# Order of VectorE's work at the group borders: turns of weights and logits ahead of the next unit's first scan

## What is computed

```python
for t in range(S):                                   # attention with a decaying state
    cur = einsum('bhd,bhe->bhde', u[None] * kt, vt)
    y[:, :, t] = einsum('bhd,bhde->bhe', rt, state + cur)
    state = wt[:, :, :, None] * state + einsum('bhd,bhe->bhde', kt, vt)

h = x @ w_in                                         # gated layer, 384 -> 2048 -> 384
x = (h * clip(h + 3, 0, 6) / 6) @ w_out

logits = x @ phi                                     # soft mixture, 32 slots, 8 experts
d = softmax of logits over the tokens;  slot_input = d.T @ x
slot_out = relu(slot_input @ w1[e]) @ w2[e]
out = (softmax of logits over the slots) @ slot_out
```

## Time and profile before

| | |
|---|---|
| median of three runs | 419.66 us (419.65 to 419.80) |
| the profiled execution's own time | 419.48 us |
| its span, first to last instruction | 417.8 us |
| granted TensorE clock, mean | 0.991 |
| PE busy | 400.4 us, 96% |
| DVE busy | 342.0 us, 82% |
| POOL busy | 187.7 us, 45% |
| ACT busy | 162.6 us, 39% |

### The profile page before, as it was taken

How to read it: one execution, slowest core, us unless ns; L and a number is a source line. 1 busy time by engine, 2 the same in 40 slices (tenths; PEclk the granted TensorE clock), 3 DMA queues, 4 the chain that set the end, 5 groups by cost and what they waited for, 6 DMA issues and landing times.

```text
span 417.8 us, 9795 instructions
## 1 busy us (share of the span) xinstructions
PE 400.4 (96%) x3913; PEld 219.5 (53%) x3913; DVE 342.0 (82%) x566; ACT 162.6 (39%) x300; POOL 187.7 (45%) x178
## 2 busy tenths in 40 slices
PE   8999999999999999999999999999999999999981
PEld 3885555555555555565554556445453444544430
DVE  7998799999998889999989998989975887662152
ACT  3586256533343245144433434351333234321141
POOL 4445988865465755445653556564450012010000
PEclk9999999999999999999999999999999999999996
DMA  8998321468033124314430321331006199779929
GB/s 246 336 404 296 125 90 36 124 238 296 17 124 119 60 70 126 91 36 124 125 108 18 123 94 41 116 123 60 0 4 249 53 352 414 251 272 410 408 106 357
DMA packets 16541, 69.35 MB, mean 166 GB/s; under 512 B 2160, under 2 KB 3184, under 8 KB 14832
## 3 DMA queue, kind: packets, MB, share of 16 engines
q1 hardware_dynamic: 16496, 68.73, 47.0%
HBM read 64.00 MB, written 4.72 MB: 164 GB/s over the span
## 4 chain that ended last, share of the span: by engine, by line
issue 36%; PE 26%; POOL 22%; DVE 7%; DMA 5%; ACT 1%; POOLq 0%; SPq 0%; DVEq 0%
POOL att L1566 5%; POOL att L1528 4%; PE hid L582 4%; POOL att L1530 4%; PE hid L584 4%; PE hid L583 4%; POOL att L1551 3%; DMA att<-rkT_dram 3%; POOL att L1584 3%; POOL w_split L1542 3%; PE hid L852 3%; PE hid L833 1%; PE sc_ps L833 1%; DVE gated L1015 1%; DVE att L922 1%
## 5 line engine op out<-in xcount | busy, mean ns | idle before, releaser
L1375 ACT ACTIVATE relu<-hid,three 128x512 f32<-128x512 f32 x95 | 65.1, 686 | 136.1 <-PE hid L584 135.6
L582 PE MATMUL hid<-x_split,w_split 128*128 128x512 f16 x285 | 108.3, 380 | 0.1
L584 PE MATMUL hid<-x_split,w_split 128*128 128x512 f16 x285 | 108.0, 379 | 0.0
L583 PE MATMUL hid<-x_split,w_split 128*128 128x512 f16 x285 | 108.0, 379 | 0.0
L1015 DVE SCALAR_TENSOR_TENSOR gated<-relu,hid 128x512 f32<-128x512 f32 x95 | 64.4, 678 | 19.9 <-ACT relu L1375 19.2
L1036 DVE STREAM_TRANSPOSE ring<-gated 128x512 f32<-128x512 f32 x96 | 68.3, 711 | 3.3
L1557 POOL TENSOR_TENSOR att<-att 128x1024 f16<-128x1024 f32 x20 | 40.9, 2045 | 48.8 <-ACT att L1308 48.8
L1575 POOL TENSOR_TENSOR att<-att 112x512 f32<-112x512 f32 x19 | 23.2, 1222 | 55.8 <-DVE att L934 55.8
L582 PEld LDWEIGHTS hid<-x_split,w_split 128*128 128x128 f16 x285 | 27.7, 97 | 36.8 <-DVE gated L1015 6.8
L584 PEld LDWEIGHTS hid<-x_split,w_split 128*128 128x128 f16 x285 | 27.8, 98 | 33.7
L583 PEld LDWEIGHTS hid<-x_split,w_split 128*128 128x128 f16 x285 | 27.9, 98 | 24.7
(11 more groups left out here) (280 smaller groups left out, 760.6 us busy)
## 6 DMA issues: line engine op xcount, KB each, us to landing
att<-nat_dram SPq DMA_DIRECT2D x20, 576.0 KB, 4.1
att<-rkT_dram SPq DMA_DIRECT2D x22, 448.0 KB, 5.5
att<-wT_dram SPq DMA_DIRECT2D x22, 226.2 KB, 4.6
att<-w_dram SPq DMA_DIRECT2D x3, 1536.0 KB, 10.3
out_dram<-w_split SPq DMA_DIRECT2D x11, 384.0 KB, 3.9
att<-w_dram SPq DMA_DIRECT2D x5, 768.0 KB, 10.8
stage<-w_in_dram SPq DMA_DIRECT2D x2, 1536.0 KB, 14.5
ring<-w_outT_dram SPq DMA_DIRECT2D x1, 3072.0 KB, 15.3
```

The source lines that it names most:

```text
L582: pe.matmul(hid[s % 2][:], high, x_high, start=(q == 0), stop=False)
L583: pe.matmul(hid[s % 2][:], high, x_low, start=False, stop=False)
L584: last = pe.matmul(hid[s % 2][:], low, x_high, start=False, stop=(q == KT - 1))
L1375: nc.scalar.activation(relu_tile(s), hid[s % 2][:], ACT.Relu, bias=three[:], scale=GATE / H_SCALE)\
```

## The change

Nothing is added or removed. In phase 1 of a step, the block that turns weights and logits moves from behind the next unit's suffix scan, its reciprocal and `low_x` to the place right behind the masking:

```diff
@@ -1178,17 +1178,17 @@
                         group_maximum(g - 1)
                     if is_unit(n):
                         mask_scores(n)
-                    if is_unit(n + 1):
-                        scan_suffix(n + 1)
-                        restart_prefix(n + 1)
-                    if is_unit(n - 1) and n % B == 0 and n > B:
-                        low_x(n - 1)
                     if 1 <= g < C and i == 2:
                         if g == C - 1:
                             turn_gated(s - 1)
                         turn_weight(g - 1)
                         if g - 1 not in idle_inc:
                             turn_logits(g - 1)
+                    if is_unit(n + 1):
+                        scan_suffix(n + 1)
+                        restart_prefix(n + 1)
+                    if is_unit(n - 1) and n % B == 0 and n > B:
+                        low_x(n - 1)
                     if g == C and i == 2:
                         last_maximum()
```

## The result

The changed kernel takes 422.39 us in the median of 22 runs, against 419.77 for the kernel before in as many: 2.6 us more, a ratio of 1.006 with a 95% interval of 1.0042 to 1.0078. It is slower, as forecast, by 0.6%. The forecast was 421.5, a loss of 1.84 against the 419.66 of the first three runs, so the loss is 1.4 times the forecast one.

A forecast was written before the change was run, and what follows sets the result against it. PE was taken to bound the kernel. Border losses 0.19 + 0.40 + 1.22 + 0 = 1.81 us on the profiled 419.48 gave 421.29; with the median 0.18 above that execution, 421.5, range 419.4 to 422.8.

The forecast's parts named there:

- Part 1: PE's gather at the borders: its wait goes, winning 0.45 us at each of borders 1 to 3, 0.5 at border 4.
- Part 2: DVE at borders 1 to 3: the scan is held by POOL's low scores, gate and all behind it 1.22 us later.
- The 1.36 and 421.9: Alternative size by the page's rule: the scan blocked in full, 1.36 us delay at each border, sum below 421.9.
- Part 3: PE behind borders: after its room, 0.19, 0.40 and 1.22 us of DVE's delay reach it at borders 1, 2, 3.
- Border 4: The scan comes first, POOL waits some 0.6 us, covered by idle time; DVE isn't moved, the 0.5 won is lost: 0.
- The scan not held: Rival at the borders: scan not held or only a little, PE wins 0.45 at borders 1 and 2; 418.8, chance 0.12.
- Cancelling: Rival: about 0.5 us hold cancels the gains, or gather waits are PE's own issue; 419.3 to 420.3, chance 0.1.
- Nothing absorbs the delay: Rival on PE behind borders: three full delays add, 3 x 1.22 = 3.7 us, 423.3; chance 0.1.
- The signs: Expected trace: scan about 2.4 us at borders 1 to 3, gather without gap, keys 1.2 later, PE idle about 1.8 more.

The follow-up runs named there:

- POOL's wait at border 1 alone: Turns ahead of the scan at border 1 alone, POOL waiting there for the scan before its low scores; 419.20 us against 419.70 for the kernel before.
- single borders: Three kernels, turns ahead of the scan only at border 1, 2 or 3: 420.10, 420.63 and 421.02 us against 419.81 for the kernel before.
- The experiment at border 4 alone: Only the weights' turn at border 4 goes ahead of the scan; 420.14 us against 419.81 for the kernel before.
- with POOL's wait: On top of the change, POOL waits for the scan before its low scores at borders 1 to 3; 420.63 us against 419.84 for the kernel before.

## Why the prediction was right or wrong

**Part 1, the gather starts earlier: right.** All four waits of the earlier trace rows are gone. What it is worth where nothing takes it back is 0.46 us at a border (the stretch with POOL's wait at border 1 alone), against 0.45 forecast.

**Part 2, the scan meets POOL: right, a little small.** Forecast 1.22 on DVE, measured 1.34. The hold itself is as forecast: the scan ends at 108.75, which without the 0.20 of the start is the forecast 108.55. An unheld one asked for at 106.31 would have ended at 107.54, so the hold is 1.21. The missing 0.12 is the order: the gate now stands right behind the reciprocal and starts 0.24 behind the scan's end (108.99 - 108.75), where I had used the 0.12 that a turn takes there. The kernel with POOL's wait at border 1 shows the same 0.25 (107.82 - 107.57) without any hold.

By the Trainium skill (SBUF — State Buffer, "Who interferes with whom") the instruction that comes first keeps the shared port pair for its whole length. The trace agrees on who waits in all cases here, both ways round. It doesn't agree on the size: the scan ended 1.09 behind POOL and not 1.23, and POOL's low scores at border 4, asked for 0.56 us before the scan's end, lost 0.36. The 1.36 and 421.9 that the prediction worked out from the page's rule lie nearer to the measured 1.34 and 422.39 than its own numbers do. That is luck: the hold is 1.21, and the rest is the order of gate and reciprocal and the two terms below, of which the rule says nothing.

**Part 3, what reaches PE: right in kind, the sizes off.** Border 1 was forecast at 0.19 and costs 0.39, border 2 at 0.40 and costs 0.74, border 3 at 1.22 and costs 1.38 (stretches of the single borders). At each border 0.12 of the difference is part 2's. A part of the rest is that a unit in which PE had to wait is followed by one of 13.15 us instead of 13.07 (140.59 - 127.44 on PE). Between unit 14 and the increment of border 3 that and a later wait make the lag grow from 1.04 to 1.21. Why, and how the last tenths split, stays open. The losses add, as forecast: 0.3 + 0.8 + 1.2 + 0.3 = 2.6 in medians.

**The wait that I overlooked** is L484 for `acc_added`. It held PE 0.4, 0.6 and 1.1 us behind the three borders. By the trace it isn't what the loss is made of: at border 3 the scores are 235.16 - 233.28 = 1.88 late and the next attention 244.86 - 242.67 = 2.19, so L999 holds PE beyond it, as forecast. But it took away part of what PE had gained before L999 did: behind border 1 the gather starts 0.53 earlier, counted from the increment, and the scores only 0.05 earlier. No run removes this wait alone.

**Border 4: wrong.** The step "POOL waits for the scan, some 0.6 us, with four idle microseconds behind its keys to cover it; DVE isn't moved" failed. The cover on POOL is there, but the delayed keys' product overlaps L1092, which I had not counted as an instruction that can be held, and DVE is moved by 0.37. The experiment at border 4 alone shows it at +0.3 to +0.4, and the 0.44 of L1092 in the trace before pointed at it. "With a late keys' product, which DVE instruction with two SBUF inputs comes next" was the question that I asked for L999 and not for L1092.

**Rivals.** The scan not held: fell. Cancelling: fell. Nothing absorbs the delay (423.3): fell, since border 1 costs 0.39 of 1.34; but the true 422.39 lies between it and the forecast.

**The signs.** The scan's 2.4 us, the gather behind the increment and the later keys came as listed, and POOL's 2.36 at border 4 near the 2.5. Units 10 and 15 show no wait in the list: the first to attend late behind border 2 is unit 14, and both it and unit 10 give themselves away only by the 0.25 to 0.26 behind L999. PE's idle time grows from 417.8 - 400.4 = 17.4 to 420.6 - 401.8 = 18.8, so by 1.4 and not by 1.8; the other half of the longer span is listed as busy.

## What to carry to other kernels

Before an instruction is moved on VectorE, list what GpSimd does in its old and in its new place, and which VectorE instructions on either side read two SBUF operands. One that was free in GpSimd's idle time can cost nearly its neighbour's remaining length in the new place (the scan: 1.21 us of 1.35), however short it is itself. Removing one collision can hand it to the next such instruction. Where one line's instruction shows two durations in the trace before, look at what GpSimd does beside the longer one: it may be held there already. Where the order can't be freed, let GpSimd wait, or fill its products' time with VectorE work that reads PSUM or a single operand; and price a delay by the room in front of the first wait that it reaches, border by border.

## What the runs showed of the hardware that I had not expected

An update of 128x1, 0.22 us by itself, stood 0.81 us (in the changed kernel) and 1.02 us (with POOL's wait) while a GpSimd product was in progress; its size didn't help it. It ended 0.01 to 0.02 us behind the product each time (284.78 and 284.76, 168.35 and 168.34). All its three operands lie in SBUF. Beside such products the turns of one SBUF operand kept 0.70 to 0.71 us, the gates (SBUF and PSUM) 0.69, and the products kept 2.00.
